# One PSUM bank per phase for the 128-feature sum, in a fused mixing and two-MLP kernel on one Trainium2 core

## The reference, cut to what matters

```python
# x (2, 4096, 192), weight_gen (2, 4096, 8 heads, 7 taps); all float32
w = softmax(weight_gen, axis=-1)
x = sum over the 7 taps k of w[..., head, k] * x_padded[position + k]     # per head of 24 features
x = x.reshape(8192, 192)
h = x @ moe_w_in          # 192 -> 2048
x = max(0.01 * h, h) @ moe_w_out      # 2048 -> 192
h = x @ moe2_w_in         # 192 -> 2048
out = where(h > 0, h, exp(min(h, 0)) - 1) @ moe2_w_out    # 2048 -> 192
```

## Time and profile before

| | |
|---|---|
| median of 3 runs | 1156.99 us (1156.66 to 1156.99) |
| the profiled execution's own time | 1156.67 us |
| its span in the profile | 1154.9 us |
| PE busy | 1133.8 us, 9804 matmuls |
| ACT, DVE, POOL busy | 750.0, 673.9, 422.4 us |
| granted TensorE clock | 0.996 of full speed in the mean |

### The profile page before, as it was taken

The page is one execution under the profiler, slowest core; times in us unless marked ns, Lnnn a source line. Parts: engine busy times, 40 slices in busy tenths (PEclk is TensorE's granted clock), DMA queues, the critical chain, the costliest instruction groups (busy, mean ns, idle before and its releaser), DMA issues.

```text
span 1154.9 us, 22749 instructions
## 1 busy us (share of the span) xinstructions
PE 1133.8 (98%) x9804; PEld 920.9 (80%) x9804; DVE 673.9 (58%) x690; ACT 750.0 (65%) x846; POOL 422.4 (37%) x409
## 2 busy tenths in 40 slices
PE   7999999999999999999999999999999999999998
PEld 4878887888878888887888878888887888888886
DVE  7766647456474655647456474564646556464554
ACT  4667758566575765757667575665657667575764
POOL 5745723608044080632707135090541806200000
PEclk9999999999999999999999999999999999999999
DMA  6313021120112102021020111101121020010000
GB/s 176 123 45 94 15 66 29 34 75 29 53 29 80 29 28 67 16 79 28 28 80 28 54 29 53 56 28 53 28 80 29 28 68 27 28 28 28 15 28 28
DMA packets 44723, 55.45 MB, mean 48 GB/s; under 512 B 4116, under 2 KB 32914, under 8 KB 44624
## 3 DMA queue, kind: packets, MB, share of 16 engines
q1 hardware_dynamic: 44624, 54.01, 15.3%
HBM read 36.29 MB, written 17.69 MB: 47 GB/s over the span
## 4 chain that ended last, share of the span: by engine, by line
PE 89%; DVE 4%; ACT 4%; issue 1%; POOL 1%; DMA 0%; SPq 0%; POOLq 0%; ACTq 0%
PE y_a_rows L614 28%; PE hidden L546 28%; PE y_b L607 19%; PE hidden L550 9%; PE hidden L575 5%; DVE hid_lo L1132 2%; DVE act L1107 2%; ACT hid_hi L920 1%; ACT act L904 1%; DMA xw<-in_x_dram 0%; ACT ya L878 0%; DVE up_b_lo L1020 0%; POOL prod L338 0%; POOL act L341 0%; POOL staged L338 0%
## 5 line engine op out<-in xcount | busy, mean ns | idle before, releaser
L614 PE MATMUL y_a_rows<-hid_hi,dn 64*128 64x512 f32 x2048 | 564.3, 386 | 0.0
L607 PE MATMUL y_b<-hid_hi,dn 64*128 64x512 f32 x1024 | 395.9, 387 | 0.5 <-PE y_b L607 0.2
L607 PE MATMUL y_b<-hid_lo,dn 64*128 64x512 f32 x1024 | 395.4, 386 | 0.0
L614 PEld LDWEIGHTS y_a_rows<-hid_hi,dn 64*128 64x128 f32 x2048 | 330.6, 184 | 39.7
L614 PE MATMUL y_a_rows<-hid_lo,dn 64*128 64x512 f32 x1024 | 353.5, 386 | 0.0
L1132 DVE TENSOR_TENSOR hid_lo<-hidden,hid_hi 128x1024 fp32r<-128x1024 f32 x128 | 156.5, 1223 | 206.6 <-ACT hid_hi L920 206.5
L1132 DVE TENSOR_TENSOR hid_lo<-act,hid_hi 128x1024 fp32r<-128x1024 f32 x127 | 172.1, 1355 | 169.7 <-ACT hid_hi L920 169.4
L902 ACT ACTIVATE hidden<-hidden 128x1024 f32<-128x1024 f32 x127 | 128.2, 1009 | 173.0 <-PE hidden L550 173.0
L314 POOL TENSOR_TENSOR mix<-xw,wk 128x384 f32<-128x384 f32 x30 | 38.8, 1294 | 549.3 <-DVE wk L1048 543.9
L904 ACT ACTIVATE act<-hidden 128x1024 f32<-128x1024 f32 x127 | 130.4, 1026 | 132.2 <-PE hidden L550 124.5
L546 PE MATMUL hidden<-in_a_hi,up_a_hi 64*128 64x512 f32 x1020 | 202.8, 394 | 8.8 <-DVE act L1107 5.6
(11 more groups left out here) (108 smaller groups left out, 1195.4 us busy)
## 6 DMA issues: line engine op xcount, KB each, us to landing
xw<-in_x_dram SPq DMA_DIRECT2D x14, 960.0 KB
raw_b<-squares_out SPq DMA_DIRECT2D x60, 96.0 KB, 2.2
out_dram<-staged SPq DMA_DIRECT2D x15, 384.0 KB, 2.6
squares_in<-prod SPq DMA_DIRECT2D x56, 96.0 KB, 2.0
squares_out<-ya SPq DMA_DIRECT2D x15, 256.0 KB, 2.1
raw_a<-squares_in SPq DMA_DIRECT2D x14, 256.0 KB, 2.7
raw_d<-in_moe_w_out_dram SPq DMA_DIRECT2D x8, 384.0 KB, 3.4
raw_a<-in_moe_w_in_dram SPq DMA_DIRECT2D x8, 256.0 KB, 3.6
```

Of the source, the lines that this page charges most:

```text
L607: return nc.tensor.matmul(y_b[:, :], dn[m][rows, f, P:2 * P], v[rows, s % HB, HALF[i]], start=start, stop=stop)
L614: return nc.tensor.matmul(bank[:, :], dn[m][rows, f, first:first + P], v[rows, s % HB, HALF[i]], start=(f == 0 and n == 0), stop=(f == FT ...
```

## The change

Each phase gets its own bank for y_a (phase mod 2) and its own bank for y_b. Low and high rows of y_a now add into the same bank, so a semaphore s_yahigh keeps the low-row matmuls behind the high-row ones of a step. Of the twelve y_a matmuls of a step, eight still pair with y_b; the four others pair with matmuls of the second up block. In the last four steps (APART) the low rows use the other bank, as before. turn is now the second y_b bank.

MLP 2's input (128 features) is read from the PSUM bank; ya is only written for MLP 2's output, by a copy in ScalarE (s_ya), and its addition in VectorE is left only at the end. The bank of phase n is written again in phase n + 2, behind s_min (the input is split) or s_ya.

Side tasks move: take_y and add_y from ahead of the activation of step 2 to behind the work of step 3; mlp2_input from steps 3, 4 to 1, 2 of the odd phases from phase 3 on; turn_mix from step 2 to 1, mlp1_input from 5, 6 to 4, 5, softmax_a from 3 to 6, softmax_b from 5 to 7, softmax_exp from 4 to 7 of the even phases.

```diff
-        y_a = [ps(f"y_a_rows{h}", [P, T]) for h in (0, 1)]
-        y_b = ps("y_b", [P, T])
-        turn = ps("turn", [P, T])
+        y_a = [ps(f"y_a{n}", [P, T]) for n in (0, 1)]
+        y_b = [ps(f"y_b{n}", [P, T]) for n in (0, 1)]
+        turn = y_b[1]
...
+            def up(m, src, g, s, second, down=None):
...
                 pe.wait_ge(s_open, g)
+                if down is not None:
+                    dm, step, d = down
+                    low(0)
+                    down_a(dm, step, d, HIGH, 1, 1)
+                    low(1)
+                    down_a(dm, step, d, HIGH, 1, 2).then_inc(s_yahigh, 1)
+                    low(2)
+                    high(0)
+                    low(3)
+                    high(1)
+
+                    pe.wait_ge(s_yahigh, d + 1)
+                    down_a(dm, step, d, LOW, 0, 0)
+                    high(2)
+                    down_a(dm, step, d, LOW, 0, 1)
+                    high(3).then_inc(s_up, 1)
+                    return
...
+            def down_open(m, s, d):
+                if s == 0 and d // ST >= 2:
+                    of, c = PHASES[d // ST - 2]
+                    pe.wait_ge(s_yb, d // ST - 1)
+                    if of == 0:
+                        pe.wait_ge(s_min, 2 * c + 1)
+                    else:
+                        pe.wait_ge(s_ya, c + 1)
...
-                down_a(m, s, HIGH, 1, 0)
-                if starts is not None:
-                    pe.wait_ge(s_ya, starts)
-                down_a(m, s, LOW, 0, 0)
-                down_a(m, s, HIGH, 1, 1)
+                down_a(m, s, d, HIGH, 1, 0)
+
+            def down_middle(m, s, d):
+                down_a(m, s, d, HIGH, 1, 1)
+                down_a(m, s, d, HIGH, 1, 2).then_inc(s_yahigh, 1)
+                pe.wait_ge(s_yahigh, d + 1)
+                down_a(m, s, d, LOW, 0, 0)
+                down_a(m, s, d, LOW, 0, 1)
+
+            def down_middle_apart(m, s, d):
+                if d == APART:
+                    pe.wait_ge(s_ya, CH - 1)
+                down_a(m, s, d, LOW, 0, 0)
+                down_a(m, s, d, HIGH, 1, 1)
+                down_a(m, s, d, LOW, 0, 1)
+                down_a(m, s, d, HIGH, 1, 2).then_inc(s_yahigh, 1)
...
+            def down_alone(m, s, d):
+                pe.wait_ge(s_lo, d + 1)
+                down_open(m, s, d)
+                if d < APART:
+                    down_middle(m, s, d)
+                else:
+                    down_middle_apart(m, s, d)
+                down_close(m, s, d)
...
                     if ph == 1 and s == 0:
-                        pe.wait_ge(s_lo, g - 2)
-                        down_open(0, ST - 3, g - 3)
-                        down_close(0, ST - 3, g - 3)
+                        down_alone(0, ST - 3, g - 3)
...
-                    if s == LAG - 1:
-                        down_close(of, step, g - LAG)
-                        up(m, input_of(m, c), g, s, True)
+                    if d < APART:
+                        up(m, input_of(m, c), g, s, True, (of, step, d))
                     else:
                         up(m, input_of(m, c), g, s, True)
-                        down_close(of, step, g - LAG)
+                        down_middle_apart(of, step, d)
+                    down_close(of, step, d)
...
-                    nc.scalar.activation(in_a_hi[input_of(1, c)][:, :], ya[0][:, :], ACT.Copy).then_inc(s_mhi, 1)
+                    nc.scalar.activation(in_a_hi[n][:, :], y_a[ph % 2][:, :], ACT.Copy).then_inc(s_mhi, 1)
...
-                    if s == LAG - 1 and dm is not None:
-                        take_y(dm, dc, ph - 1)
                     activation(m, c, g, s)
...
                         exponential(c, s)
+                    if s == LAG and dm is not None:
+                        take_y(dm, dc, ph - 1)
...
-                    if m == 1 and s in (5, 6) and not (known(c) and c >= CH - 2):
-                        mlp1_input_hi(c + 2, s - 5)
-                    if m == 0 and s in (3, 4) and not (known(c) and c == 0):
-                        mlp2_input_hi(c - 1, s - 3)
+                    if m == 1 and s in (4, 5) and c < CH - 2:
+                        mlp1_input_hi(c + 2, s - 4)
+                    if ph == 1 and s in (3, 4):
+                        mlp2_input_hi(0, s - 3)
+                    if m == 0 and c > 1 and s in (1, 2):
+                        mlp2_input_hi(c - 1, s - 1)
...
-                    if m == 1 and s == 4 and not (known(c) and c >= CH - 3):
+                    if m == 1 and s == 7 and c < CH - 3:
                         softmax_exp(c + 3)
```

More of the change, by code:

```diff
@@ L206, in attention_leaky_elu_mlps @@
         LAST = 2 * CH - 1
+        PHASES = [(0, 0), (0, 1), (1, 0)]
+        for n in range(2, CH):
+            PHASES += [(0, n), (1, n - 1)]
+        PHASES += [(1, CH - 1)]
         def input_of(m, c):
@@ L606, in down_b, with down_a @@
                 start, stop = f == 0 and n == 0 and rows == LOW, f == FT - 1 and n == 1 and rows == HIGH
-                return nc.tensor.matmul(y_b[:, :], dn[m][rows, f, P:2 * P], v[rows, s % HB, HALF[i]], start=start, stop=stop)
-            def down_a(m, s, rows, i, n):
+                return nc.tensor.matmul(y_b[d // ST % 2][:, :], dn[m][rows, f, P:2 * P], v[rows, s % HB, HALF[i]], start=start, stop=stop)
+            def down_a(m, s, d, rows, i, n):
                 f = 2 * s + i
[L612 to L615, removed]
@@ new lines, in down_a @@
+                bank, start, stop = d // ST % 2, f == 0 and n == 0 and rows == HIGH, f == FT - 1 and n == 2
+                if d < APART:
+                    stop = stop and rows == LOW
+                elif rows == LOW:
+                    bank, start = 1 - bank, d == APART and i == 0 and n == 0
+                return nc.tensor.matmul(y_a[bank][:, :], dn[m][rows, f, w:w + P], v[rows, s % HB, HALF[i]], start=start, stop=stop)
+            def down_open(m, s, d):
[6 more added lines that the diff above has]
+                        pe.wait_ge(s_ya, c + 1)
+                if d:
+                    pe.wait_ge(s_dn, d)
+                down_b(m, s, d, LOW, 0, 0)
+                down_a(m, s, d, HIGH, 0, 0)
+                down_b(m, s, d, LOW, 0, 1)
+                down_a(m, s, d, HIGH, 0, 1)
+                down_b(m, s, d, LOW, 1, 0)
+                down_a(m, s, d, HIGH, 0, 2)
+                down_b(m, s, d, LOW, 1, 1).then_inc(s_yblow, 1)
+                down_a(m, s, d, HIGH, 1, 0)
@@ L844, in mlp2_input_hi @@
             def mlp2_input_hi(c, part):
+                ph = phase_mlp1(c) if c else 0
+                n = input_of(1, c)
                 if part == 0:
[L847 to L850 removed]
+                    act_e.wait_ge(s_dn, ST * (ph + 1))
+                    if c in (0, CH - 1):
                         act_e.wait_ge(s_up, ST * (ph + 1))
@@ L861, in take_y @@
+                    nc.scalar.activation(in_b_up[n][D2:P, :], yb[0][:, :], ACT.Copy)
+                    nc.scalar.activation(in_b[n][0:D2, :], yb[0][:, :], ACT.Copy).then_inc(s_mhi, 1)
             def take_y(dm, dc, ph):
-                last = known(ph) and ph == LAST
                 def copy_low():
                     act_e.wait_ge(s_dn, ST * (ph + 1))
-                    if not (known(ph) and ph == 0):
+                    if ph:
                         act_e.wait_ge(s_yb, ph)
-                    nc.scalar.activation(ylow[:, :], y_b[D2:P, :], ACT.Copy).then_inc(s_ylow, 1)
@@ L871, in copy_a @@
-                def copy_a():
-                    if not (known(dc) and dc == 0):
-                        act_e.wait_ge(s_outw if dm else s_min, 32 * dc if dm else 2 * dc)
-                    dst, src = ya[dm][:, :], y_a[1][:, :]
-                    if last:
-                        dst, src = last_columns(dst, True), last_columns(src, False)
-                    nc.scalar.activation(dst, src, ACT.Copy).then_inc(s_ya1, 1)
-                if last:
+                    nc.scalar.activation(ylow[:, :], y_b[ph % 2][D2:P, :], ACT.Copy).then_inc(s_ylow, 1)
@@ L1062, in mlp2_input_lo @@
                 n = input_of(1, c)
+                ph = phase_mlp1(c) if c else 0
                 dve.wait_ge(s_mhi, 2 * c + 1 + part)
                 if part == 0:
-                    nc.vector.tensor_tensor(in_a_lo[n][:, :], ya[0][:, :], in_a_hi[n][:, :].bitcast(f32), ALU.subtract).then_inc(s_min, 1)
+                    nc.vector.tensor_tensor(in_a_lo[n][:, :], y_a[ph % 2][:, :], in_a_hi[n][:, :].bitcast(f32), ALU.subtract).then_inc(s_min, 1)
                 else:
@@ L1144, in phase @@
                         mlp1_input_lo(1, 1)
-                    if s == LAG - 1 and dm is not None:
-                        add_y(dm, dc, ph - 1)
                     if s == 0 and dm == 1:
@@ L1158, in phase @@
                         softmax_b(2)
-                    if m == 1 and s == 2 and not (known(c) and c >= CH - 2):
+                    if s == LAG and dm is not None:
+                        add_y(dm, dc, ph - 1)
```

(1 more changed line is left out.)

178 lines of the change are left out of this document (83 added, 95 removed).

## The result

The changed kernel took 1143.01 us in the median of 4 runs (1141.91 to 1143.96), the kernel before 1156.99 (4 runs, 1156.66 to 1157.21). The ratio is 0.988 with a 95% interval of 0.9865 to 0.9895. Run once more beside an experiment it gave 1142.52 and 0.9874 (0.9859 to 0.9888). So it is 1.2% faster, where 1.0% was forecast (1145.0); the range was 1142.5 to 1151.5. The profiled execution took 1143.43 us with a span of 1141.4: 13.24 us less than the profiled one before, and 13.5 less in the span.

A forecast was written before the change was run, and what follows sets the result against it. PE, busy 98% of the span, bounds the kernel, so only holes in its stream count: 1156.67 - 10.2 - 3.5 + 0.7 + 1.0 = 1144.7, said as 1145.0 us because the median is 0.3 higher; range 1142.5 to 1151.5.

The forecast's parts named there:

- Slots: PE's stream: a slot is one matmul pair, 0.227 us; 19 a step before and after, 4.31 us, so 0 change.
- The 16 holes of 0.64: Step 3 to 4, even phases 2 to 30 and phase 31: later take_y makes step 2 ordinary, 10.2 us back.
- The 13 holes of 0.27: Last step of even phases 2 to 26: in_b ready a step earlier, 3.5 us back.
- MLP 2's input from PSUM: 16 copies and 16 additions of ya leave ScalarE and VectorE, which lie beside PE: worth nothing.
- The wait on s_yahigh: Mixed block, 250 times: 0.56 us needed, 0.68 allowed, spare 0.12; taken as 0, upper bound 12.5 us.
- The rival (slower by a biting wait): Mixed block: the s_yahigh wait bites, kernel not faster; at worst 0.064 us a step, 1161 us; chance 0.12.
- The first layer's start: Step 0 of odd phases: hid_lo one slot later but less held by GpSimd; 0.05 a time, 0.7 us lost.
- the rival's 3.5: Odd phases: hid_lo still meets a full GpSimd instruction, 0.25 late 14 times, 3.5 us; 1147.8 us, chance 0.18.
- Start of the kernel: Phase 1: 1.6 us lost, 0.9 back, 0.3 lost; together +1.0 us, bounds 0 and 2.4.
- The two lone blocks: Phase 1: two down blocks run alone with four unpaired matmuls each and the new wait bare; 1.6 us lost.
- VectorE's crowding in phase 1: Phase 1: VectorE gets add_y in the step in which weights are split; 0.3 us lost.
- the port term: Odd phases' step 0: hid_lo waiting for GpSimd on the port pair shared with VectorE; 0.7 us lost, bounds 0 and 3.5.

The follow-up runs named there:

- the two copy experiments: Changed kernel with take_y and add_y back ahead of step 2's activation: 1168.08 us; kernel before with take_y behind that activation, one set of banks: 1199.56 us.

## Why the prediction was right, point by point

*Slots.* 19 a step before and after: 4.31 stayed. Shown by all kernels but those that shorten the room for the wait or use up the slack.

*The 16 holes of 0.64.* 10.2 us forecast; all 16 steps are 4.30 or 4.31 now. That the late copies bring it, and that they need both the second bank set and the step behind the Relu, is shown by the two copy experiments, one in each kernel. The prediction named the copies and the late up block together; the weights, 0.21 and 1.13 of 1.34 us, came out only with the Relu at 3.60.

*The 13 holes of 0.27.* 3.5 us forecast. Shown twice: taken away in the kernel before, put back alone in the changed one (3.5, in 14 phases). The prediction puts it down to the place of the copies; 0.25 of it was GpSimd beside in_b, as phase 28 shows, so the softmax's move alone should have repaired most of it.

*MLP 2's input from PSUM.* The work that leaves was costed at nothing; shown by putting it back.

*The wait on s_yahigh.* Costed at nothing with a spare of 0.12 us. Nothing it was. The spare is smaller than the prediction's: the price curve of 0.127 and 0.373 a step at one slot and none puts the need at 0.58 to 0.60 us from start to start, against three slots, 0.68, so 0.08 to 0.10. The rival (slower by a biting wait) was one slot away: 31 us, and the kernel would have been 1.5% slower than before.

*The first layer's start.* Here a term was mis-sized. The prediction took 0.05 a time, 0.7 us; it cost 0, and the 4.33 of before went as well, 0.3 more. The mechanism was right: hid_lo meets the rest of one product only. But it was to be held 0.4 there, giving back 0.3, and it was held 0.23 and gave back 0.46, so the next one ends at 7.29 against 7.48 allowed. With the softmax in its old place 2.5 us of the rival's 3.5 appear, in 13 phases and not 14.

*Start of the kernel.* The two lone blocks cost 1.13 + 0.43 = 1.56 (1.6 forecast), the earlier s_up of step 1 gave 0.91 back (0.9 forecast). The 0.3 for VectorE's crowding in phase 1 did not come: its steps there stay at 4.33 or less.

*The sum.* Forecast -12.0 for the profiled execution, measured -13.24. Between the hand at step 0 of phase 2 and step 7 of phase 31 the time fell from 1135.67 - 91.83 = 1043.84 to 1121.97 - 92.68 = 1029.29, 14.55 us, against 13.0 in the forecast. Of the 1.55 difference 0.7 is the port term; 0.4 stood in 18 steps of 4.33 or 4.34; 0.15 is that the holes are 0.642 and 0.275 each; and 0.3 stood in steps of 4.31 to 4.32, most of them behind the holes. The second profile of the changed kernel has the same 1029.29, so this is no scatter: the forecast was short by small terms that it rounded away or charged for nothing.

The front lost 0.85 (forecast 1.0), but 0.20 of it lies ahead of the first hand, which stands anywhere from 22.99 to 24.12 in the twelve profiles. Behind the last hand the changed kernel's span has 19.4 us in one profile and 18.6 in the other, before 19.2, so nothing can be read from the tail. The medians of the changed kernel are 1143.01 and 1142.52: 2.0 and 2.5 below the forecast, and the second stands at the very low end of the range.

## What to carry to other kernels

When an engine with a fixed order stream is full, look at the distance between two like instructions step by step: a handful of steps that differ name all that can be won, and each hole's price times its count sums up to the result. A second accumulator bank is worth what its evacuation may then be late, not the bandwidth; spread side tasks into measured room and not into the step where they become possible. Before a same-engine wait goes into a full stream, measure the latency at a place where it stands bare, and put at least that much independent work between.

## What the runs showed that I had not expected

The margin is small, and beyond it every missing slot is paid in full. Two slots between signal and wait cost nothing, one costs 31 us and none 92 us. After such a restart the next five pairs came 0.232 us apart instead of 0.227, which makes a fifth of the price in the kernel with one slot; what slows them is not settled. And VectorE's delay by GpSimd depends on the moment of meeting and not on load: the same hid_lo took 1.23 alone and 1.46, 1.87 or 1.92 us as more of the GpSimd instruction was left.
